# Linear attention in front of a mixture of experts: key-values computed with the features stationary

## The reference

```python
def phi(x):
    proj = np.einsum('bhsd,df->bhsf', x, w_phi)
    proj = proj - np.max(np.abs(proj), axis=-1, keepdims=True)
    return np.concatenate([np.exp(proj), np.exp(-proj)], axis=-1)
q_p, k_p = (phi(q), phi(k))
kv = np.einsum('bhsf,bhsd->bhfd', k_p, v)
z = np.sum(k_p, axis=2)
num = np.einsum('bhsf,bhfd->bhsd', q_p, kv)
den = np.einsum('bhsf,bhf->bhs', q_p, z)[..., None] + 1e-06
return (num / den).astype(np.float32)
```

## Time and profile before

| | us |
|---|---|
| runs (3) | 884.08, 884.13, 885.58; median 884.13 |
| profiled execution: device time | 885.49 |
| profiled execution: span | 883.5 |
| PE busy | 866.3 (98%) |
| PE weight loads busy | 784.7 (89%) |
| DVE, ACT, POOL busy | 559.8, 433.4, 297.7 |

### The profile page before, as it was taken

How to read it: one execution, slowest core, us unless ns; L and a number is a source line. 1 busy time by engine, 2 the same in 40 slices (tenths; PEclk the granted TensorE clock), 3 DMA queues, 4 the chain that set the end, 5 groups by cost and what they waited for, 6 DMA issues and landing times.

```text
span 883.5 us, 20242 instructions
## 1 busy us (share of the span) xinstructions
PE 866.3 (98%) x7394; PEld 784.7 (89%) x7395; DVE 559.8 (63%) x837; ACT 433.4 (49%) x793; POOL 297.7 (34%) x264
## 2 busy tenths in 40 slices
PE   7999999979999999999999999999999999999997
PEld 5888888878888888888888899999999999999997
DVE  4777777798704799930470145642668998778882
ACT  5666666543433444334434557655666743333430
POOL 5687776624434555544452210000000011111111
PEclk9999999989999999999999999999999999999999
DMA  5555555316713578561111047745467644444421
GB/s 163 149 163 155 157 163 155 116 47 215 244 49 113 179 254 261 166 173 48 65 48 36 13 116 183 191 121 141 115 195 206 191 150 138 134 130 121 141 73 48
DMA packets 126679, 122.04 MB, mean 138 GB/s; under 512 B 35040, under 2 KB 101728, under 8 KB 126624
## 3 DMA queue, kind: packets, MB, share of 16 engines
q1 hardware_dynamic: 119088, 103.15, 40.0%
q0 software_dynamic: 3504, 11.28, 3.9%
q10 hardware_dynamic: 4032, 6.86, 2.1%
HBM read 86.39 MB, written 34.88 MB: 137 GB/s over the span
## 4 chain that ended last, share of the span: by engine, by line
PE 94%; DVE 2%; SPq 1%; POOL 1%; DMA 1%; issue 0%; ACT 0%; POOLq 0%; DVEq 0%
PE bank L731 24%; PE bank L729 24%; PE bank L730 24%; PE bank L806 4%; PE bank L745 4%; PE bank L759 3%; PE bank L964 3%; PE bank L724 2%; PE bank L786 1%; PE bank L934 1%; PE bank L1003 1%; PE bank L779 1%; PE bank L908 1%; PE bank L768 1%; PE bank L762 1%
## 5 line engine op out<-in xcount | busy, mean ns | idle before, releaser
L712 POOL DMA_INDIRECT out<-temps,ids x18 | 25.1, 1395 | 323.8 <-DVE temps L1653 321.3
L684 POOL TENSOR_TENSOR h_lo<-h_raw,h_hi 128x512 fp32r<-128x512 f32 x49 | 76.7, 1585 | 126.4 <-ACT h_hi L1221 126.4
L729 PE MATMUL bank<-ops,place 128*128 128x384 f32 (+1 forms) x357 | 119.1, 334 | 0.0
L731 PE MATMUL bank<-ops,place 128*128 128x384 f32 (+1 forms) x357 | 118.3, 331 | 0.0
L730 PE MATMUL bank<-ops,place 128*128 128x384 f32 (+1 forms) x357 | 118.3, 331 | 0.0
L1715 DVE TENSOR_TENSOR temps<-temps,bank 128x384 f32<-128x384 f32 x72 | 39.7, 553 | 73.9 <-PE bank L731 73.8
L729 PE MATMUL bank<-place,ops 128*128 128x256 f32 x294 | 83.2, 283 | 0.0
L730 PE MATMUL bank<-place,ops 128*128 128x256 f32 x294 | 83.2, 283 | 0.0
L731 PE MATMUL bank<-place,ops 128*128 128x256 f32 x294 | 83.2, 283 | 0.0
L1624 DVE CAST w_hi<-ahead 128x1024 fp32r<-128x1024 f32 x48 | 52.3, 1091 | 45.2 <-PE bank L731 45.0
L729 PE MATMUL bank<-w_hi,h_hi 128*128 x200 | 80.4, 402 | 0.2 <-issue 0.2
(11 more groups left out here) (251 smaller groups left out, 2160.1 us busy)
## 6 DMA issues: line engine op xcount, KB each, us to landing
ahead<-in_moe_w SPq DMA_DIRECT2D x56, 512.0 KB, 4.6
h_rows<-temps SPq DMA_DIRECT2D x96, 192.0 KB, 2.5
w_raw<-h_rows SPq DMA_DIRECT2D x17, 512.0 KB, 3.8
y_sorted<-y ACTq DMA_DIRECT2D x25, 256.5 KB, 3.0
raw<-h_rows SPq DMA_DIRECT2D x10, 512.0 KB, 3.7
tail<-h_rows SPq DMA_DIRECT2D x9, 512.0 KB, 3.7
qk<-in_k SPq DMA_DIRECT2D x16, 256.0 KB, 4.5
vs<-in_v SPq DMA_DIRECT2D x16, 256.0 KB, 2.9
```

The lines of the kernel that those rows point to most:

```text
L684: nc.gpsimd.tensor_tensor(h_lo[:, fs, :], h_raw[:, fs, :], h_hi[:, fs, :].bitcast(F32), ALU.subtract).then_inc(h_lo_done, 1)
L729: mm(o, left_hi, right_hi, start=first, stop=False, skip_group_check=shared)
L731: return mm(o, left_lo, right_hi, start=False, stop=last, skip_group_check=shared)
```

## The change

In the new kernel the key features are stationary (two halves of 64 features, twice for exp and exp(-x)) and the values are moving, 65 columns: the 64 values and a column of ones, which yields the sum of the features. The result has features on partitions at once, so the sums on GpSimd, `key_sums`, `z_ones` and `z_pick` go. Only the gate numbers still need the key-values with the head dimension on partitions: DVE copies the bank to `kv`, with the numbers of the two batch entries interleaved by column (`[P, 2, DX, 2]`); PE transposes 128 such columns twice (`transpose_kv`); ACT copies that; and two matmuls of 32 columns give the gate numbers of both entries (`gates_by_feature`), which ACT adds to `kv` (`move_gates`). The numerators read 81 columns of `kv`, which now lie 8 bytes apart. `kv` has two buffers.

The values land in `v_raw`, and GpSimd copies them into the 65 column layout. The mixed slot of keys, and that of queries, is loaded by one transfer and not two, and the mixed slot of the output is stored by one.

```diff
+    DV = DH + 1
+    DX = DV + GATES + 1
+    KVT, KVG = 0, 3 * P
-                    for b in range(2):
-                        sp.dma_start(qk[par][64 * b:64 * (b + 1), mix, :], rows[b, QS * P:S, :]).then_inc(qk_loaded[par], 16)
+                    sp.dma_start(qk[par][:, mix, :], rows[:, QS * P:S, :]).then_inc(qk_loaded[par], 16)
...
-            def sum_slots(g):
...
+            def copy_values(g):
+
+                pool.wait_ge(v_loaded[g % 2], 16 * (g // 2 + 1))
+                if g >= 2:
+                    pool.wait_ge(kv_done, g - 1)
+                nc.gpsimd.tensor_copy(vs[g % 2][:, :, 0:DH], v_raw[g % 2][:]).then_inc(v_copied, 1)
...
             for g in range(GROUPS):
                 if g < GROUPS - 1:
-                    sum_slots(g + 1)
+                    add_logits(g)
+                if g + 2 < GROUPS:
+                    copy_values(g + 2)
                 if g % 2 == 0:
                     split_chunk(g // 2)
...
-                if g < GROUPS - 1:
-                    add_logits(g)
...
                 for j in range(QS):
                     for b in range(2):
-                        mm(bank[64 * b:64 * (b + 1), ps_kv, 0:2 * F], vs[par][:, QS * b + j, :], phi_k[par][:, QS * b + j, :, :],
-                           start=(j == 0), stop=False)
+                        for c in range(2):
+                            for m in halves:
+                                at = (2 * c + b) * DV
+                                mm(bank[m, ps_kv, at:at + DV], phi_k[par][:, QS * b + j, c, m], vs[par][:, QS * b + j, :],
+                                   start=(j == 0 and b == 0 and c == 0), stop=False, skip_group_check=True)
+                for c in range(2):
+                    for m in halves:
+                        last = mm(bank[m, ps_kv, 2 * c * DV:2 * (c + 1) * DV], phi_k[par][:, K_MIX, c, m],
+                                  v_mix[par][:].rearrange("p b d -> p (b d)"), start=False, stop=True, skip_group_check=True)
+                last.then_inc(kv_done, 1)
+
+            def transpose_kv(g, par):
+
+                pe.wait_ge(kv_copied, g + 1)
+                for c in range(2):
+                    last = tr(bank[:, ps_kv, KVT + c * F:KVT + (c + 1) * F],
+                              kv[par][:, c, 0:DH, :].rearrange("p d b -> p (d b)"), ident[:])
                 last.then_inc(kvT_done, 1)
 
-            def key_values_by_feature(g):
+            def gates_by_feature(g):
 
                 pe.wait_ge(kvT_moved, g + 1)
...
+                    at = KVG + 2 * GATES * c
+                    last = mm(bank[:, ps_kv, at:at + 2 * GATES], kvT[:, c, :],
+                              w_head[:, ds(g % H, 1), :, :].rearrange("p a b e -> p (a b e)"), start=True, stop=True)
+                last.then_inc(gates_done, 1)
...
-                                      query_place(par, s // PER_UNIT)[:, s % PER_UNIT, c, 64 * m:64 * (m + 1)], kv[:, c, b if s else m, 0:DEN + 1],
+                                      query_place(par, s // PER_UNIT)[:, s % PER_UNIT, c, 64 * m:64 * (m + 1)], kv[par][:, c, 0:DV + GATES, b if s else m],
```

On ACT, `move_kvT` moves from between the two `key_features` to the end of a group, behind `query_features(g, par, 1)`, and `move_gates(g - 1)` comes behind the first two `move_pairs`. On DVE the copy of the key-values (`copy_kv`) moves ahead of the second `normalize`, and in the last group ahead of `choose(0)`:

```diff
                 if nxt:
                     shift(n, npar, 1)
+                if cur:
+                    copy_kv(g, par)
                 if cur and not nxt:
                     choose(0)
                 if prev:
                     normalize(g - 1, 1, npar)
-                if cur:
-                    move_kv(g)
                 if cur and not nxt:
                     place_first_half()
```

More of the change, by code:

```diff
@@ L115, in build_attention_moe_ffn @@
         qk = [alloc(region, f"qk{i}", [P, 2 * SLOTS, DH]) for i in range(2)]
-        vs = [alloc(region, f"vs{i}", [P, 2 * QS, DH]) for i in range(2)]
-        v_mix = [alloc(region, f"v_mix{i}", [P, 2, DH]) for i in range(2)]
-        kvz = alloc(region, "kvz", [P, 2, 2 * F])
-        z_pairs = alloc(region, "z_pairs", [P, 2, 2, 2 * F])
-        z_sum = alloc(region, "z_sum", [P, 2, 2 * F])
-        kv = alloc(region, "kv", [P, 2, 2, DX])
+        vs = [alloc(region, f"vs{i}", [P, 2 * QS, DV]) for i in range(2)]
+        v_raw = [alloc(region, f"v_raw{i}", [P, 2 * QS, DH]) for i in range(2)]
+        v_mix = [alloc(region, f"v_mix{i}", [P, 2, DV]) for i in range(2)]
+        kvT = alloc(region, "kvT", [P, 2, F])
+        kv = [alloc(region, f"kv{i}", [P, 2, DX, 2]) for i in range(2)]
         mx = [alloc(region, f"mx{i}", [P, 2, PER_UNIT]) for i in range(2)]
@@ L299, in build_attention_moe_ffn @@
         v_loaded = [sem(f"v_loaded{i}") for i in range(2)]
+        v_mix_loaded = [sem(f"v_mix_loaded{i}") for i in range(2)]
+        v_copied = sem("v_copied")
         stage_loaded = [sem(f"stage_loaded{i}") for i in range(2)]
@@ L382, in load_v @@
                 rows = vh[r:r + H + 1:H, :, :]
-                sp.dma_start(vs[par][:, 0:2 * QS, :].rearrange("p (b j) d -> p b (j d)", b=2),
+                if isinstance(g, int) and g < 2:
+                    sp.wait_ge(v_ones, g + 1)
+                sp.dma_start(v_raw[par][:, 0:2 * QS, :].rearrange("p (b j) d -> p b (j d)", b=2),
                              rows[:, 0:QS * P, :].rearrange("b (p j) d -> p b (j d)", j=QS)).then_inc(v_loaded[par], 16)
                 for b in range(2):
-                    sp.dma_start(v_mix[par][64 * b:64 * (b + 1), b, :], rows[b, QS * P:S, :]).then_inc(v_loaded[par], 16)
+                    sp.dma_start(v_mix[par][64 * b:64 * (b + 1), b, 0:DH], rows[b, QS * P:S, :]).then_inc(v_mix_loaded[par], 16)
             def store_x(g):
@@ L395, in store_x @@
                                  xg[g % 2][:, at:at + QS, :]).then_inc(x_stored[g % 2], 16)
-                    sp.dma_start(x_tok[first + QS * P:first + S, cols],
-                                 xg[g % 2][64 * b:64 * (b + 1), QS, :]).then_inc(x_stored[g % 2], 16)
+                both = x_tok[2 * (g // H) * S:2 * (g // H + 1) * S, cols].rearrange("(b t) d -> b t d", b=2)
+                sp.dma_start(both[:, QS * P:S, :], xg[g % 2][:, QS, :]).then_inc(x_stored[g % 2], 16)
             def load_group(g, par, qk_there=False):
@@ L828, in attention @@
                 n, npar = g + 1, 1 - par
+                if prev and not nxt:
+                    gates_by_feature(g - 1)
                 if nxt:
@@ L836, in attention @@
                     transpose_pairs(n, npar, 0)
+                    if prev:
+                        gates_by_feature(g - 1)
                     if isinstance(n, int) and n == 0:
-                        pe.wait_ge(qk_loaded[0], 5 * 16)
-                    if not (isinstance(g, int) and g <= 0):
-                        pe.wait_ge(kv_moved, g)
+                        pe.wait_ge(qk_loaded[0], 3 * 16)
                     transpose_pairs(n, npar, 1)
@@ L881, in attention @@
                         rank_first_half()
+                        gates_by_feature(g)
                 if nxt:
@@ L1133, in move_kvT, with move_gates @@
                 act.wait_ge(kvT_done, g + 1)
-                nc.scalar.copy(kvz[:], bank[:, ps_kv, :].rearrange("p (a n) -> p a n", a=2)).then_inc(kvT_moved, 1)
+                nc.scalar.copy(kvT[:], bank[:, ps_kv, KVT:KVT + 2 * F].rearrange("p (c f) -> p c f", c=2)).then_inc(kvT_moved, 1)
+            def move_gates(g, par):
+                act.wait_ge(gates_done, g + 1)
+                nc.scalar.copy(kv[par][:, :, DV:DV + GATES, :],
+                               bank[:, ps_kv, KVG:KVG + 4 * GATES].rearrange("p (c b e) -> p c e b", c=2, b=2)).then_inc(kv_ready, 1)
             def key_features(n, npar, u):
@@ L1155, in attention @@
                     move_pairs(n, 1)
+                if prev:
+                    move_gates(g - 1, npar)
                 if cur and nxt:
@@ L1165, in attention @@
                     key_features(n, npar, 0)
-                if cur:
-                    move_kvT(g)
-                if nxt:
                     key_features(n, npar, 1)
@@ L1173, in attention @@
                     query_features(g, par, 1)
+                    move_kvT(g)
                 if cur and not nxt:
                     query_features(g, par, 2)
+                    move_gates(g, par)
             src, at, mix = Q_PART
@@ L1180, in _ @@
                           rows0[:, 0:QS * P, :].rearrange("b (p j) d -> p b (j d)", j=QS)).then_inc(qk_loaded[0], 16)
-            for b in range(2):
-                act.dma_start(qk[0][64 * b:64 * (b + 1), mix, :], rows0[b, QS * P:S, :]).then_inc(qk_loaded[0], 16)
+            act.dma_start(qk[0][:, mix, :], rows0[:, QS * P:S, :]).then_inc(qk_loaded[0], 16)
             attention(-1, 1, cur=False, prev=False)
```

103 lines of the change are left out of this document (32 added, 71 removed).

## The result

The kernel with the change takes 890.01 us (median of 4 runs, 888.90 to 891.54), the kernel before, on the same chip, 884.86: a ratio of 1.0059, interval 1.0046 to 1.0072. The forecast was 877.3 with a range up to 883.6. The change makes the kernel slower by 0.6%. Two executions in all, one of `e8_unrolled` (949.3 us) and one of the kernel before beside e5 to e8 (1732.4 us), are far slower than the rest and aren't counted.

What follows compares the result with a forecast made beforehand. PE was taken to bound attention. 885.49 - 6.3 (steady part) - 1.9 (start) + 2.4 (last group) - 1.0 (clock) = 878.7 us profiled, 877.3 against the median; own range 873 to 881, with ends and rivals 1 and 2, 871.5 to 883.6.

Steps and rivals of the forecast that it cites:

- PE has 0.57 less to do in a period: Attention's steady part: 3.57 us of PE work goes, 3.00 comes; after 0.12 of waiting, 0.45 per period, 6.3 us over 14.
- The numerators read 81 columns 8 bytes apart ... I take nothing: Numerators in attention: the 8 byte step costs nothing, with an upper price of 3.3 us per group, 53 us over 16.
- Rival 3: Numerators: the 8 byte step costs, up to 53 us; decides from 17% on a record, 930 at full price; chance 0.07.
- SP loses three issues of about 0.6 per group, which hides behind PE: SP's transfer queue during attention: three fewer issues of about 0.6 us per group, hidden behind PE.
- The start: Group 0: 1.4 us gained up to the projection, 0.5 from one issue less; together 1.9, between 0.5 and 2.6.
- The last group: Group 15: `normalize` 1.9 us later behind GpSimd's split, numerators 0.5 later; together 2.4 lost, between 1.0 and 4.0.
- The clock: Tail behind the ranking: longer PE pauses bring the low clock earlier, fillers run faster; 1.0 us gained, 0.5 lost to 2.2 gained.
- The ends of the range: Steady part's extremes: 0.77 a period (10.8 us) gained at best, -1.0 us at the dearest gates.
- Rivals 1, 2 and 4: 1: key-values 36.3 ns a record (0.14); 2: ACT's chain takes PE's place (0.10); 4: loading bounds short matmuls, 897 (0.04).
- Rival 5: Tail: the low clock stays through the fillers and first expert tile, 3 to 4 us more, 881; chance 0.05.
- three signs of being wrong: Period over 10.6 us, PE waiting on ACT over 0.3 in it, or ranking not later relative to the last key-values.

Runs made afterwards that it cites:

- e8_unrolled: Changed kernel with the loads of keys and queries split, plus PE's code for groups 2 and 3 written out ahead of its loop; 886.74 us, ratio 1.0020.
- e5: Changed kernel with the loads of keys and queries split, plus a second copy of the key-values, columns side by side, for the numerators; 882.70 us, ratio 0.9969.
- e9: e7 with e5's second copy of the key-values for the numerators; 877.92 us, ratio 0.9908.
- e3: Kernel before with only the merged loads of the mixed slots of keys and queries; 891.07 us, ratio 1.0067.
- e2: Changed kernel with the mixed slots' loads and stores all split again, as in the kernel before; 892.12 us, ratio 1.0073.
- e6: Changed kernel, transfers still merged, with SyncE issuing keys and queries ahead of stores and values, and weights' chunks behind them; 883.18 us, ratio 0.9984.
- e4: e2 with GpSimd splitting the eighth chunk of weights ahead of its wait for group 14's logits; 888.99 us, ratio 1.0042.
- e15: Kernel before with both of PE's tail pauses filled: 40 fillers ahead of the one-hots, 82 behind the ranks; 884.41 us, ratio 0.9983.
- e13: e9 with 82 instead of 48 fillers behind the ranks, closing PE's second tail pause, the first left open; 876.94 us, ratio 0.9900.
- e7: Changed kernel with the loads of keys and queries split, plus GpSimd's order of e4 and SyncE's order of e6; 880.19 us, ratio 0.9939.

## Why the prediction failed, by its own steps

- *"PE has 0.57 less to do in a period"*: nearly right in e9's form, 0.43 less with no wait. In the change as it is, four pieces were off. The key-values took 29 ns a record and not 31 (0.12 less). The gates took 0.36 and not 0.28. From the transposes to the projection passed 0.50, where the working had 0.41 with its wait. The fourth is the next point. The period without a wait is 10.50, not 10.32.
- *"The numerators read 81 columns 8 bytes apart ... I take nothing"*: 0.17 a group, 2.4 us over the 14 periods, shown by e5. Rival 3 had the mechanism, and its own bound says that at 3.6 ns a record it doesn't decide. The reason given was float32's slow stream. The Trainium skill, "SBUF — State Buffer", note on cachelines, gives full bandwidth to two hits in a line of 16 bytes, by which the step was free as well; the measurement says 6%.
- *"SP loses three issues of about 0.6 per group, which hides behind PE"*: this is the step that failed. Fewer issues did not mean sooner data. The loads had 0.2 us to spare, which the same queue would have told: in the kernel before SyncE's round opens with the stores at 95.12, the queries' last transfer is issued at 103.5 and lands at 107.1, and PE asks at 107.29. PE's shorter period and the merged transfer's 2.3 us more ate it in every second group, where two chunks of weights stand ahead. The six periods with a wait are 6.3 us too long together, 4.9 of it in the waits themselves, and no rival had it. e3 shows the merged loads on the kernel before alone, e2 that PE's sooner asking is enough without them, e6 that the place in the queue decides.
- *The start*: -1.9 was forecast, +0.5 came. At the start of group 0's key-values the changed kernel is 1.9 later (15.95 for 14.05), where 0.5 was to be gained. The second set of transposes starts 0.87 later, behind the merged transfer of the keys. The other 1.0 comes of the slow pace of PE there, which the change didn't bring: as far as the traces tell it is chance. From there to the mark pass 4.75 for 6.18, 1.4 less, as was kept, and that with the stall of 0.71 in it. In e9, whose records are not slow and which has no such stall, the mark is at 18.83, again 1.4 earlier than before. The 0.5 for an issue less didn't come in either.
- *The last group*: +2.4 forecast, +2.8 measured, by the instructions named (`normalize` at 10.79 for 10.75). The other 0.4 is in how much later behind the last projection group 15's key-values start (4.21 for 3.33, 0.9 where 0.5 was taken).
- *The clock*: the sign was right, the size 2.25 for 1.0, and the reason isn't borne out. It was to be the longer pauses, but e3 and e4, whose first pause is 2.3 as before, have the same fast 80 fillers (4.65). In the changed kernel the low level came in the first pause and was over before those fillers; whether it does differs between kernels in a way that no run explains. To that extent the term was luck.
- *The ends of the range* were added wrongly. With 1.90 for the key-values and no wait the terms give 0.65 a period and not 0.77, 9.1 us and not 10.8; at 2.32, the dearest gates and 0.2 of waits more they give -0.35 and so -4.9 us, not -1.0. The forecast itself isn't touched.
- *Rivals 1, 2 and 4* are dead: 29 ns a record, and 0.2 us of waits on ACT in 14 periods. Rival 5 didn't come: the clock was at 1.00 again from 199 us on. Of the three signs of being wrong, one came, the period (10.98 on average, over 10.6); the ranking is later, 13.9 behind the last key-values where it was 12.2.

The span is 10.5 us longer than forecast, and these make 10.4 of it: 6.6 in delayed periods (the 6.3, and 0.3 in the first period), 2.5 in the period itself, 2.4 at the start, 0.4 in the last group, less 1.5 in the tail.

## What to carry to other kernels

Before you merge transfers, look at what becomes the outermost dimension, and add up the queue: from the start of a round to the issue of the transfer that is needed, plus its landing, against the time at which the engine asks for it. If that sum is near, an engine that is idle by its busy share is the next bound, and making the bounding engine faster calls it. Put the loads first and the stores behind them; in e6 that removed all such waits, and PE got no new wait on another engine for it.

The version with all four repairs (loads split and issued first, GpSimd's split early, a second copy laid out for the numerators) and the tail's pauses closed takes 876.8 us, 0.9% less than the kernel before. The kernel before with its pauses closed as well has 0.2% of that (e15). The rest is mostly PE's shorter period, 10.34 against 10.77, 6.0 us over 14, so the reformulation is worth it and what came with it was not. Whether the loads issued first would have given the kernel before something at its start wasn't run.

## What I had not expected of the hardware

- A transfer of 32 KB whose pattern begins with a dimension of 2 landed in 5.97 us, with a DMA share of 0.15 over the last 2 us; as two transfers of 16 KB each, issued one behind the other, the last landed in 3.69 (e2).
- A float32 moving operand that takes every second element costs 2.4 ns more per record of 81 columns, on 36 ns, so 6 to 7%.
- A pause of TensorE of 2.05 us, with another of 2.3 ahead of it or with that one filled, was followed by 3 to 7 us at the 1.2 GHz level. 34 more fillers in it kept the clock at 1.00, even with the first pause left (e13). In e7 the clock fell with no such pause, so this isn't all.
- The first 48 records of the projection, 7 us into the trace, take 1.55 us in most traces and 2.77 in six of the 18, also where the code up to there is the same (e9, e13). Two single traces can differ by over 1 us for this alone.
- TensorE stalls without a releaser, 0.3 to 2.2 us long and all ahead of 50 us, stand in 11 of the 14 profiled kernels with the 64 short matmuls a group, and in none of the 4 with the matmuls of before. Their size changes from kernel to kernel by over 1 us, and their cause stays open.
